# Attention's second pass: two steps of the state in one round of the tensor engine's loop

## What is computed

```python
batch, n_heads, seq, head_dim = (4, 8, 768, 40)
for t in range(S):
    y[:, :, t] = np.einsum('bhd,bhde->bhe', rt, state)
    Sa = np.einsum('bhde,bhe->bhd', state, at)
    state = state * wt[:, :, None, :] - np.einsum('bhd,bhe->bhde', Sa, bt)
    state = state + np.einsum('bhd,bhe->bhde', vt, kt)
```

## Time and profile before

| | us |
|---|---|
| three runs | 1095.31, 1093.55, 1095.19 |
| median | 1095.19 |
| the profiled execution | 1087.87 |
| its span, first to last instruction | 1086.1 |
| first pass | 0 to 141.8 |
| second pass | 141.8 to 384.2 |
| routing of tokens | 384.2 to 408 |
| experts | 408 to 705 |
| dense layer | 705 to 1086.1 |

### The profile page before, as it was taken

The page is one execution under the profiler, slowest core; times in us unless marked ns, Lnnn a source line. Parts: engine busy times, 40 slices in busy tenths (PEclk is TensorE's granted clock), DMA queues, the critical chain, the costliest instruction groups (busy, mean ns, idle before and its releaser), DMA issues. The chain is left out here.

```text
span 1086.1 us, 47433 instructions
## 1 busy us (share of the span) xinstructions
PE 971.8 (89%) x21169; PEld 851.9 (78%) x21170; DVE 605.9 (56%) x968; ACT 318.7 (29%) x739; POOL 284.7 (26%) x349
## 2 busy tenths in 40 slices
PE   3426779999998989999999999979999999999997
PEld 3425768888888848888878888849999989999896
DVE  8997959888887661112211111146656566666664
ACT  5525646655555500000000000031221222222211
POOL 1008989898800003116601100060101000000000
PEclk9999989899999998999999999989999999999999
DMA  7877757878887438997885544330010101010101
GB/s 232 231 178 209 230 164 240 241 237 258 241 243 247 138 121 268 303 288 239 243 271 180 152 162 151 106 91 13 25 25 25 25 1 25 1 25 1 26 1 25
DMA packets 119984, 159.61 MB, mean 147 GB/s; under 512 B 60164, under 2 KB 91028, under 8 KB 119540
## 3 DMA queue, kind: packets, MB, share of 16 engines
q1 hardware_dynamic: 109636, 128.46, 38.6%
q0 software_dynamic: 5824, 25.28, 7.8%
q10 hardware_dynamic: 4464, 5.08, 1.3%
HBM read 133.15 MB, written 19.23 MB: 140 GB/s over the span
## 5 line engine op out<-in xcount | busy, mean ns | idle before, releaser
L1068 DVE TENSOR_SCALAR ht<-h_bank 128x512 f32<-128x512 f32 x62 | 42.9, 692 | 238.4 <-PE h_bank L1045 238.4
L1305 ACT CAST g_hi<-g 128x512 fp32r<-128x512 f32 x96 | 59.5, 620 | 280.2 <-DVE g L1263 280.2
L1056 PE MATMUL y_bank<-w_all,ht 128*128 x496 | 138.6, 433 | 0.0
L1193 PE MATMUL y_bank<-w_out_hi,g_hi 128*128 128x320 f32 x384 | 119.4, 311 | 2.5 <-DVE g_lo L1243 2.5
L1045 PE MATMUL h_bank<-xt,w 128*128 128x128 f32 x992 | 121.0, 281 | 0.0
L1056 PEld LDWEIGHTS y_bank<-w_all,ht 128*128 128x128 f32 x496 | 91.8, 190 | 34.3
L1193 PE MATMUL y_bank<-w_out_hi,g_lo 128*128 128x320 f32 x384 | 118.7, 309 | 0.0
L1193 PE MATMUL y_bank<-w_out_lo,g_hi 128*128 128x320 f32 x384 | 118.5, 309 | 0.0
L1045 PEld LDWEIGHTS h_bank<-xt,w 128*128 128x128 f32 x992 | 115.0, 194 | 3.9 <-issue 0.2
L1180 PE MATMUL h_bank<-xt_hi,w_in_hi 128*128 128x512 f32 x288 | 114.6, 398 | 1.3 <-DVE xt_hi L1226 1.3
L1180 PE MATMUL h_bank<-xt_hi,w_in_lo 128*128 128x512 f32 x288 | 113.4, 394 | 0.0
(11 more groups left out here) (187 smaller groups left out, 1747.1 us busy)
## 6 DMA issues: line engine op xcount, KB each, us to landing
w<-w_in SPq DMA_DIRECT2D x31, 1024.0 KB, 6.0
t_in<-wab_in SPq DMA_DIRECT2D x24, 776.0 KB, 6.4
t_in<-wak_in SPq DMA_DIRECT2D x24, 776.0 KB, 5.8
w_all<-w_in POOLq DMA_DIRECT2D x8, 1280.0 KB, 9.8
rr<-rr_in SPq DMA_DIRECT2D x24, 384.0 KB, 3.3
w_rest<-w_in SPq DMA_DIRECT2D x62, 128.0 KB, 3.7
vt<-vt_in SPq DMA_DIRECT2D x24, 256.0 KB, 3.4
vtm<-vtm_in SPq DMA_DIRECT2D x24, 240.0 KB
```

The source lines that it names most:

```text
L1056: last = pe.matmul(y_bank[s][:, 0:FEAT], ht[s][:, f, :], w2[:, ds(e * W2 + f * FEAT, FEAT)], start=f == 0, stop=f == NF - 1)
L1068: dve.tensor_scalar(ht[s][:, FH * n:FH * n + FH, :].rearrange("q f t -> q (f t)"), h_bank[s][n][:, :], 0.0, None, ALU.max).then_inc(s_relu, 1)
L1193: last = pe.matmul(y_bank[n][:, 0:FEAT], g_part[j % RING][:, n * PARTS:(n + 1) * PARTS], v[:, f, :], start=f == 0 and p == 0, stop=f == NF ...
L1305: act.copy(g_hi[j % RING][:, :], g[j % 2][:, :]).then_inc(s_ghi, 1)
```

## The change

The loop of the second pass on PE runs twelve rounds, and its body holds two steps, s = 0 and s = 1. The step's number is k = 2 i + (s - 1), and each wait that had the count i has k, the one that had i + 1 has 2 i + s, and the two with multiples have 96 i + 48 (s - 1) and 64 i + 32 (s - 1): the same counts in the same order. The products, their order and the other engines' code are the same.

```diff
@@ -885,42 +885,44 @@
-            with pe.Fori(1, STEPS + 1) as i:
-                arrive(s_ax_vtm, 48 * i)
-                arrive(out_of["st"], i)
-                heads(alpha_s, BA, DIM, closes=False)
-                arrive(out_of["g2"], i)
-                heads(g2_v, BA, DIM, opens=False, done="w")
...
-                arrive(s_vt_rr, 32 * i)
...
-                arrive(out_of["st"], i + 1)
-                picks()
-                arrive(out_of["m2"], i)
-                heads(from_b(lambda i, q, m: m2[rows(m), slot(q, i), :]), BB, C, opens=False, done="y")
+            with pe.Fori(1, STEPS // 2 + 1) as i:
+                for s in two:
+                    k = 2 * i + (s - 1)
+                    arrive(s_ax_vtm, 96 * i + 48 * (s - 1))
+                    arrive(out_of["st"], k)
+                    heads(alpha_s, BA, DIM, closes=False)
+                    arrive(out_of["g2"], k)
+                    heads(g2_v, BA, DIM, opens=False, done="w")
...
+                    arrive(s_vt_rr, 64 * i + 32 * (s - 1))
...
+                    arrive(out_of["st"], 2 * i + s)
+                    picks()
+                    arrive(out_of["m2"], k)
+                    heads(from_b(lambda i, q, m: m2[rows(m), slot(q, i), :]), BB, C, opens=False, done="y")
```

More of the change, by code:

```diff
@@ new lines, in _ @@
+            with pe.Fori(1, STEPS // 2 + 1) as i:
[6 more added lines that the diff above has]
+                    heads(g2_v, BA, DIM, opens=False, done="w")
+                    arrive(out_of["y"], k)
+                    heads(turned_state, BB, DIM, done="s")
+                    arrive(out_of["pick"], k)
+                    heads(turned(second), BD, DIM, done="ktm")
+                    arrive(out_of["w"], k)
+                    heads(u_product, BC, DIM, done="u")
+                    arrive(out_of["s"], k)
+                    arrive(out_of["ktm"], k)
+                    heads(from_s(lambda i, q, m: eye(m)), BD, DIM, closes=False)
+                    heads(from_k(lambda i, q, m: at_m(vtm, i, q, m, rows(m))), BD, DIM, opens=False, closes=False)
+                    arrive(out_of["u"], k)
+                    heads(low_part, BA, DIM, done="z")
+                    arrive(s_vt_rr, 64 * i + 32 * (s - 1))
+                    heads(m1_product, BB, C, done="m1")
+                    arrive(out_of["z"], k)
+                    heads(sa_product, BC, DIM, done="sa")
+                    heads(sat_product, BA, C, done="sat")
+                    arrive(out_of["m1"], k)
+                    heads(from_s(lambda i, q, m: at_m(rr, i, q, m, live(m))), BB, C, closes=False)
+                    arrive(out_of["sa"], k)
+                    heads(from_b(lambda i, q, m: sa_tm[rows(m), slot(q ^ m, i), :]), BD, DIM, opens=False, done="st")
+                    arrive(out_of["sat"], k)
+                    heads(m2_product, BA, C, done="m2")
+                    arrive(s_alpha, k)
+                    heads(with_alpha(second), BC, C, done="g2")
+                    heads(from_k(lambda i, q, m: m1[rows(m), slot(q, i), :]), BB, C, opens=False, closes=False)
+                    arrive(out_of["st"], 2 * i + s)
+                    picks()
+                    arrive(out_of["m2"], k)
+                    heads(from_b(lambda i, q, m: m2[rows(m), slot(q, i), :]), BB, C, opens=False, done="y")
```

## The result

The changed kernel takes 1353.16 us, median of four runs (1349.57 to 1356.13), against 1094.37 us before (four runs, one more than the table of the kernel before has): a ratio of 1.2388, 95% interval 1.2337 to 1.2438. It is 259 us slower. The forecast was 1369 us, range 1245 to 1450.

The account below looks back on a forecast made before the run. The tensor engine was taken to bound the second pass. With ten blocks fetched again each round, 42.0 + 433 + 38.6 + about 3 us made 516.6 us against 242.3: +274 us, 1369 us, range 1245 to 1450.

Parts of the forecast that it names:

- What bounds, and the blocks: Second pass of attention: the tensor engine bounds it; the loop body grows from five 256-instruction blocks to ten.
- The store's size: Tensor engine's instruction store: the trace shows seven blocks kept at most; ten would not fit, chance 0.84.
- case A: Second-pass loop: store under ten blocks, oldest dropped first, all fetched again each round; 1369 us (1303 to 1458), chance 0.66.
- case B: Second-pass loop: store too small, but a block displaces only the one at its own place; about 1265 us, chance 0.18.
- The sum: Second pass with all blocks fetched again each round: 516.6 us against 242.3, +274 us.
- the edge: End of a loop round, its target block missing from the store: 5.5 us, ends 4.5 and 7.5.
- The choice of the price by the DMA load: Each block not in the store: 4.2 us, ends 3.7 and 4.83, chosen for DMA engines busy some 0.35.
- The stalls: Tensor engine's timeline in the second pass: a stall on "issue" of 2 us every 126 matmuls.
- The packets: Instruction queue q8, whole execution: 36 packets before, 150 to 160 after if all blocks are fetched again.
- The gain of 2.2 us: Twelve of the second-pass loop's 24 branches removed: 2.2 us gained, 4.4 at most, 0 at least.
- The arithmetic: Computed wait counts on the tensor engine's sequencer: taken as 0, 21 us in the pass if uncovered, very unlikely.
- Case C: Second-pass loop: store holds everything, the second step is new code once at 8.0 us; 1101 us (1097 to 1106), chance 0.11.

## Why the prediction was right

**What bounds, and the blocks: right.** Five blocks before, ten after, and the stalls stand where the counting put them.

**The store's size: right, and now shown.** The prediction could take from the trace only that seven blocks are kept, and gave 0.84 to a store too small for ten. The runs with 7 and 8 blocks of body put it at eight. The Trainium skill ("Runtime: NRT & Kernel Launch", "Instruction fetch mechanics") gives 128 KiB, which come to eight blocks, and the runs agree; with its statement that there are only two lines they don't.

**Which block is dropped: case A, right.** Eleven packets in a round, all ten blocks and the one ahead; case B had six. The runs of 8 blocks show the order: nine a round, or two and seven in turn.

**The sum: 516.6 us for the pass, 508.1 measured; +274 against +265.8.** Term by term: round 1 42.0, measured 43.0; rounds 2 to 11 433, measured 611.20 - 182.75 = 428.5; round 12 38.6, measured 36.6; the block behind the loop 3, measured none (PE waits 0.85 us for `yt` there, and waited 1.01 us before). Within a round two errors met: from 182.75 to 218.46 us nine blocks took 3.97 us each where I took 4.2, and the edge 6.83 us where I took 5.5; that they nearly cancel is luck. The 6.9 us that the prediction named for an edge at which the block ahead is fetched first were nearer. The choice of the price by the DMA load came out: a share of 0.39 against an expected 0.35, and the price is that of the quiet stretch. No run changes that load alone, so that it sets the price isn't shown. The low end, 3.7 us, was not low enough: 3.45 us is seen in the run with 11 added products.

**The stalls: their size was wrong, and a mechanism was left out.** I expected about 2 us every 126 matmuls. Most are 0.2 to 1.9 us. The clock fell to 0.56 and PE's own work filled the difference: at 0.57, 126 matmuls keep PE busy for 3.5 us of the 4 that a fetch takes, so the lower clock costs little beside the fetches here. One block of the round shows it: from 214.38 to 218.46 us the clock was 0.89 and PE's work 2.38 us, and the block took 4.08 us all the same; from 206.47 to 210.73, at 0.50 with 3.46 us of work, 4.26 us. I had seen the 0.57 and used it as a floor alone.

**The packets: 150 to 160 said, 161 measured.**

**The gain of 2.2 us: not seen, and not measured by itself.** A second edge costs some 0.4 us where it shows, which fits its size. **The arithmetic: taken at nothing, and costs 0.12 us at an edge**; over 24 steps with 17 waits each all of it came to 0 to 6 us, so the upper end of 21 us was far off.

**Case C's price, 8 us for a second new step, may be too low**: 13 us measured (5 to 22). The lower clock can go on into the step behind; how much of the 13 us that is stays open.

**One reading of the trace was incomplete.** The prediction says that what the steps take over 9.44 us is seen in their waits. The step from 208.70 us on takes 11.70 us with 0.29 us of waiting behind it; the rest is its clock, 0.71. The forecast didn't hang on it.

## What to carry to other kernels

Before a loop's body is written out twice, count its instructions on each engine against the largest loop that the trace shows with no fetches: past the store's size the whole body is fetched again in every round, and here three products too many cost 493 us, where all 24 branches together are worth 24 x 0.29 = 7 us. Look at the queue of instruction packets in a stretch of warm rounds; it must be silent. Near the limit count blocks and not instructions, the one ahead included, since code put in front of a loop can push it over.

## What the runs showed of the hardware

The tensor engine keeps eight blocks of 256 instructions: a body in seven runs with no fetch, one in eight with nine fetches a round. One block is asked for ahead, and it takes a place. A block comes in 3.45 to 4.8 us. I hadn't expected these. By the packets, the request isn't made where little of a last block that has just come is run (61 or some 90 instructions; with 121 it is), which with 61 gave rounds of 19 and 26 us in turn; that is an inference from counts of packets. A semaphore increment of PE alone costs 0.155 us at most. And a step whose code is in the store can run at the lower clock: 14.2 us instead of 9.44 behind stalls, at 0.54, and 12.6 us behind a single wait of 1.94 us, at 0.59.
